# Four experts' expansions on one core: Strassen's scheme for two slices, two blocks of d_model and two halves of a tile's tokens

## The reference

```python
def _moe2_ref(x, domain_probs, w1, w2):      # x 1536 x 384, w1 4 x 384 x 1024, w2 4 x 1024 x 384
    p = domain_probs / (domain_probs.sum(-1, keepdims=True) + 1e-09)
    out = np.zeros((N, D), dtype=np.float32)
    for e in range(E):
        h = np.maximum(x @ w1[e], 0.0)
        out += p[:, e:e + 1] * (h @ w2[e])
    return out
```

## Time and profile before

| | |
|---|---|
| median of 3 runs | 681.5 us (680.98 to 681.69) |
| profiled execution | 681.51 us, span 679.7 us |
| granted TensorE clock | 1.0 of full |
| TensorE busy | 670.0 us (99%) |
| VectorE, ScalarE, GpSimd busy | 267.6, 182.4, 163.1 us |
| expert stage, from the first relu to the last matmul's start | 271.35 to 675.62 us |

### The profile page before, as it was taken

One profiled execution on the slowest core, in us unless ns is written; L12 is line 12 of the kernel. 1 busy time (PEld: TensorE's weight loads), 2 busy tenths in 40 slices (PEclk: granted clock), 3 DMA queues, 4 the chain that ended last, 5 costly groups with the idle time before them and its releaser, 6 DMA issues.

```text
span 679.7 us, 10802 instructions
## 1 busy us (share of the span) xinstructions
PE 670.0 (99%) x4251; PEld 589.1 (87%) x4251; DVE 267.6 (39%) x462; ACT 182.4 (27%) x351; POOL 163.1 (24%) x173
## 2 busy tenths in 40 slices
PE   9999999999999999999999999999999999999997
PEld 6888899877778888899999999999999999999997
DVE  7888878765634333212121212121212121212122
ACT  3663444433435444211111111111111111111110
POOL 3888322222001666400025400026300000000000
PEclk9999999999999999999999999999999999999999
DMA  9913322220001332100013100013100000001011
GB/s 342 405 60 124 118 83 87 79 82 1 1 1 42 96 96 94 46 1 1 0 47 94 47 0 0 0 47 95 45 1 0 0 1 0 1 1 46 0 47 47
DMA packets 12857, 38.74 MB, mean 57 GB/s; under 512 B 1552, under 2 KB 3344, under 8 KB 12816
## 3 DMA queue, kind: packets, MB, share of 16 engines
q1 hardware_dynamic: 12528, 37.77, 16.2%
q10 hardware_dynamic: 288, 0.39, 0.2%
HBM read 35.80 MB, written 2.36 MB: 56 GB/s over the span
## 4 chain that ended last, share of the span: by engine, by line
PE 91%; DVE 5%; ACT 1%; issue 1%; POOL 1%; DVEq 0%; ACTq 0%; POOLq 0%
PE bank L909 29%; PE bank L911 28%; PE bank L910 28%; PE bank L799 2%; PE bank L878 1%; DVE fr L546 1%; PE bank L856 1%; DVE fr L538 1%; PE bank L825 1%; DVE w_lo L630 1%; PE bank L811 1%; PE bank L868 1%; DVE bank L665 0%; DVE x_lo L622 0%; DVE g_lo L671 0%
## 5 line engine op out<-in xcount | busy, mean ns | idle before, releaser
L742 DVE SCALAR_TENSOR_TENSOR g_lo<-bank,g_hi 128x512 fp32r<-128x512 f32 x96 | 66.4, 692 | 308.4 <-ACT g_hi L506 308.4
L909 PE MATMUL bank<-x_lo,w_hi 128*128 128x512 f32 (+2 forms) x480 | 182.0, 379 | 1.7 <-DVE x_lo L622 0.9
L911 PE MATMUL bank<-x_hi,w_hi 128*128 128x512 f32 (+2 forms) x480 | 178.6, 372 | 0.0
L910 PE MATMUL bank<-x_hi,w_lo 128*128 128x512 f32 (+2 forms) x480 | 177.3, 369 | 0.0
L506 ACT ACTIVATE g_hi<-bank 128x512 fp32r<-128x512 f32 x96 | 57.5, 599 | 340.9 <-PE bank L911 340.9
L911 PE MATMUL bank<-w_hi,g_hi 128*128 128x384 f32 x384 | 129.7, 338 | 0.0
L910 PE MATMUL bank<-w_hi,g_lo 128*128 128x384 f32 x384 | 129.6, 337 | 0.0
L909 PE MATMUL bank<-w_lo,g_hi 128*128 128x384 f32 x384 | 129.3, 337 | 0.0
L911 PEld LDWEIGHTS bank<-x_hi,w_hi 128*128 128x128 f32 x480 | 90.1, 188 | 17.6
L909 PEld LDWEIGHTS bank<-x_lo,w_hi 128*128 128x128 f32 x480 | 90.1, 188 | 17.2 <-issue 1.8
L910 PEld LDWEIGHTS bank<-x_hi,w_lo 128*128 128x128 f32 x480 | 90.3, 188 | 12.7
(11 more groups left out here) (71 smaller groups left out, 545.4 us busy)
## 6 DMA issues: line engine op xcount, KB each, us to landing
raw<-w_dram SPq DMA_DIRECT2D x48, 384.0 KB, 3.1
rkw<-rkw_dram SPq DMA_DIRECT2D x10, 772.5 KB, 4.4
tok<-tok_dram SPq DMA_DIRECT2D x12, 576.0 KB, 4.2
out_dram<-acc SPq DMA_DIRECT2D x10, 192.0 KB, 1.9
rkw<-rkw_dram SPq DMA_DIRECT2D x2, 512.0 KB, 4.4
rkw<-rkw_dram SPq DMA_DIRECT2D x2, 260.5 KB, 3.4
out_dram<-acc ACTq DMA_DIRECT2D x2, 192.0 KB, 2.3
u_rep<-u_dram SPq DMA_DIRECT2D x1, 192.0 KB, 6.2
```

The source lines that it names most:

```text
L742: dve.scalar_tensor_tensor(out=g2[1][:, r, :], in0=p_h[j % 2][:, :], scalar=0.0, in1=g2[0][:, r, :].bitcast(F32), op0=ALU.max, op1=ALU.sub ...
L909: pe.matmul(out, wh, ml, start=start, stop=False)
L910: pe.matmul(out, wl, mh, start=False, stop=False)
L911: return pe.matmul(out, wh, mh, start=False, stop=stop)
```

## The change

A pair of slices (hidden rows 1 and 2) by the first two of three blocks of d_model, times those two blocks of x by two halves of 256 tokens, is a 2 x 2 by 2 x 2 block product. It is now computed with seven block products in place of eight (Winograd's form), of the blocks and of sums of them on either side. The third block of d_model is added as before, over all 512 tokens.

- **TensorE** (`up2`, per pair): P1 and P6 into the halves of bank 6, P7 and P5 into those of bank 7, then the third block's product for both slices into banks 0 and 1, onto which the last three products are added: two on bank 0 (one a half) and one on the first half of bank 1. `down_pair` contracts both slices of the pair before.
- **ScalarE** copies P1 and P5 to SBUF (`copy_products`) ahead of the pair's two relus.
- **VectorE** (`combine`) adds up what the four blocks of the result need, in banks 0 and 1, ahead of the two lo parts.
- **GpSimd** forms four sums of weight blocks for each pair (`split`) and four sums of x's blocks for each tile, once (`token_sums`), and splits them all into hi and lo parts.
- **Space**: slots 0 to 3 of the weights' arrays hold the sums of six pairs, slots 4 to 15 six pairs of slices (before: eight pairs). `acc` and `g2` move to where the first stage's arrays lie; the sums of tokens and copies get room behind them.

Lines that only open semaphores and some waits are left out, as are unchanged lines.

```diff
@@ -54,6 +54,14 @@
+QUARTER = TILE // 2
+PAIRS2 = J2 // 2
+NPAIR = NE * PAIRS2
+SUMS = 4
+FREE = SUMS * P * 6 // (2 * DM)
+RING2 = (J1 - FREE) // 2
@@ -138,9 +146,15 @@
-            sb("beside_g1", [P, 2 * TILE + 2 * RING1 * TILE], scope=scope)
...
+            xt_hi = sb("xt_hi", [P, NT * SUMS * QUARTER], F32R, scope=scope)
+            with ExitStack() as inner:
+                xt_raw = sb("xt_raw", [P, NT * SUMS * QUARTER], scope=inner)
+            xt_lo = sb("xt_lo", [P, NT * SUMS * QUARTER], F32R, scope=scope)
+            x_whole = sb("x_whole", [P, 2, 2, QUARTER], scope=scope)
+            u_sum = sb("u_sum", [P, 3, QUARTER], scope=scope)
+            p_copy = sb("p_copy", [P, 2, QUARTER], scope=scope)
@@ -235,7 +256,11 @@
         def slot_of(e, j):
-            return e % 2 * J2 + j
+            return FREE + (e * PAIRS2 + j // 2) % RING2 * 2 + j % 2
+        def sums_of(t, g):
+            return t[:, 0:FREE, :].rearrange("p s c -> p (s c)")[:, g % RING2 * SUMS * P:(g % RING2 + 1) * SUMS * P]
@@ -287,11 +312,11 @@
             def load_expert_slice(e, j):
-                slot = slot_of(e, j)
-                if e < 2:
+                slot, used = slot_of(e, j), e * PAIRS2 + j // 2 - RING2
+                if used < 0:
...
-                    sp.wait_ge(s_down, STEP1 + (e - 1) * (NT * J2) - J2 + j + 1 + RING)
+                    sp.wait_ge(s_down, STEP1 + used // PAIRS2 * (NT * J2) + (NT - 1) * J2 + used % PAIRS2 * 2 + 2 + RING)
...
@@ -380,14 +405,57 @@
-            def split(e, j):
-                slot = slot_of(e, j)
-                pool.wait_ge(s_raw[slot], 16 * (e // 2 + 2))
-                pool.tensor_copy(w_hi[:, slot, :], raw[:, slot, :]).then_inc(s_wp, 1)
-                pool.wait_ge(s_wp, e * J2 + j + 1)
-                pool.tensor_tensor(w_lo[:, slot, :], raw[:, slot, :], w_hi[:, slot, :].bitcast(F32),
+            def split(g):
+                e, q = g // PAIRS2, g % PAIRS2
+                slots = slot_of(e, 2 * q), slot_of(e, 2 * q + 1)
+                for slot in slots:
+                    pool.wait_ge(s_raw[slot], 16 * (g // RING2 + 2))
+                a11, a12 = raw[:, slots[0], 0:P], raw[:, slots[0], P:2 * P]
+                a21, a22 = raw[:, slots[1], 0:P], raw[:, slots[1], P:2 * P]
+                s1, s2, s3, s4 = (sums_of(raw, g)[:, i * P:(i + 1) * P] for i in range(SUMS))
+                pool.tensor_tensor(s1, a21, a22, ALU.add).then_inc(s_ws, 1)
+                pool.tensor_tensor(s3, a11, a21, ALU.subtract).then_inc(s_ws, 1)
...
+                pool.tensor_tensor(s2, s1, a11, ALU.subtract).then_inc(s_ws, 1)
...
+                pool.tensor_tensor(s4, a12, s2, ALU.subtract).then_inc(s_ws, 1)
+                for slot in slots:
+                    pool.tensor_copy(w_hi[:, slot, :], raw[:, slot, :]).then_inc(s_wp, 1)
...
+                pool.tensor_copy(sums_of(w_hi, g), sums_of(raw, g)).then_inc(s_wp, 1)
+                for i, slot in enumerate(slots):
...
+                    pool.tensor_tensor(w_lo[:, slot, :], raw[:, slot, :], w_hi[:, slot, :].bitcast(F32),
+                                       ALU.subtract).then_inc(s_w, 1)
...
+                pool.tensor_tensor(sums_of(w_lo, g), sums_of(raw, g), sums_of(w_hi, g).bitcast(F32),
...
+            def token_sums(T):
+                pool.wait_ge(s_py, NC)
+                pool.wait_ge(s_x2, KT + (T + 2) * KT)
+                cols = slice(T * TILE, (T + 1) * TILE)
+                for k in range(2):
+                    pool.tensor_tensor(x_whole[:, k, :, :].rearrange("p h t -> p (h t)"), x_hi[:, k, cols].bitcast(F32),
+                                       x_lo[:, k, cols].bitcast(F32), ALU.add).then_inc(s_xq, 1)
+                first = T * SUMS * QUARTER
+                t1, t2, t3, t4 = (xt_raw[:, first + i * QUARTER:first + (i + 1) * QUARTER] for i in range(SUMS))
...
+                pool.tensor_tensor(t1, x_whole[:, 0, 1, :], x_whole[:, 0, 0, :], ALU.subtract).then_inc(s_xq, 1)
...
+                pool.tensor_tensor(t3, x_whole[:, 1, 1, :], x_whole[:, 0, 1, :], ALU.subtract).then_inc(s_xq, 1)
...
+                pool.tensor_tensor(t2, x_whole[:, 1, 1, :], t1, ALU.subtract).then_inc(s_xq, 1)
...
+                pool.tensor_tensor(t4, x_whole[:, 1, 0, :], t2, ALU.subtract).then_inc(s_xq, 1)
...
+                sums = slice(first, first + SUMS * QUARTER)
+                pool.tensor_copy(xt_hi[:, sums], xt_raw[:, sums]).then_inc(s_xq, 1)
...
+                pool.tensor_tensor(xt_lo[:, sums], xt_raw[:, sums], xt_hi[:, sums].bitcast(F32),
+                                   ALU.subtract).then_inc(s_xt, 1)
@@ -417,9 +485,15 @@
-            for e in range(NE):
-                for j in range(J2):
-                    split(e, j)
+            token_sums(0)
+            for g in range(PAIRS2):
+                split(g)
+            token_sums(1)
+            for g in range(PAIRS2, RING2):
+                split(g)
+            token_sums(2)
+            for g in range(RING2, NPAIR):
+                split(g)
@@ -500,20 +574,36 @@
-            def hi_relu(n, j):
-                act.wait_ge(s_up, n + 1)
-                act.wait_ge(s_down, n + 1)
-                act.activation(g2[0][:, j % RING, :], p_h[j % 2][:, :], ACT.Relu).then_inc(s_gh, 1)
-            for j in range(LAG):
-                hi_relu(STEP1 + j, j)
+            def hi_relu(i, p, o):
+                act.wait_ge(s_c, i * 4 + 2 * o + 2)
+                act.wait_ge(s_down, i * 2 + (STEP1 + o + 1))
+                act.activation(g2[0][:, p % 2 * 2 + o, :], bank[o][:, :], ACT.Relu).then_inc(s_gh, 1)
+            def copy_products(i):
+                act.wait_ge(s_p, i * 4 + 1)
+                need(act, s_c, i * 4 - 3)
+                act.copy(p_copy[:, 0, :], bank[6][:, 0:QUARTER]).then_inc(s_pc, 1)
+                act.wait_ge(s_p, i * 4 + 2)
+                need(act, s_c, i * 4 - 1)
+                act.copy(p_copy[:, 1, :], bank[7][:, QUARTER:TILE]).then_inc(s_pc, 1)
+            def pair(i, p):
+                copy_products(i)
+                for o in range(2):
+                    hi_relu(i, p, o)
+            pair(0, 0)
             for m in range(KT):
...
-            for j in range(LAG, J2):
-                hi_relu(STEP1 + j, j)
+            for p in range(1, PAIRS2):
+                pair(p, p)
...
-                for j in range(J2):
-                    hi_relu(it * J2 + (STEP1 + j), j)
+                for p in range(PAIRS2):
+                    pair(it * PAIRS2 + p, p)
@@ -736,12 +826,41 @@
-            def lo_relu(n, j):
-                r = j % RING
-                dve.wait_ge(s_gh, n + (1 - STEP1))
-                dve.scalar_tensor_tensor(out=g2[1][:, r, :], in0=p_h[j % 2][:, :], scalar=0.0,
-                                         in1=g2[0][:, r, :].bitcast(F32), op0=ALU.max,
-                                         op1=ALU.subtract).then_inc(s_g, 1)
+            def combine(i):
+                p1, p5 = (p_copy[:, k, :] for k in range(2))
+                p6 = bank[6][:, QUARTER:TILE]
+                c11, c12, c22 = bank[0][:, 0:QUARTER], bank[0][:, QUARTER:TILE], bank[1][:, QUARTER:TILE]
+                u2, u3, u4 = (u_sum[:, k, :] for k in range(3))
+                def twice(ap):
+                    return ap.unsqueeze(1).broadcast_to([P, 2, QUARTER])
+                def in_halves(ap):
+                    return ap.rearrange("p (h t) -> p h t", h=2)
+                dve.wait_ge(s_pc, i * 2 + 1)
+                dve.tensor_tensor(u2, p1, p6, ALU.add).then_inc(s_u2, 1)
+                dve.wait_ge(s_pc, i * 2 + 2)
+                dve.wait_ge(s_u2, i * 2 + 1)
+                dve.tensor_tensor(u_sum[:, 1:3, :], in_halves(bank[7][:, :]), twice(u2), ALU.add).then_inc(s_u2, 1)
+                dve.wait_ge(s_p, i * 4 + 3)
+                dve.tensor_tensor(c11, p1, c11, ALU.add).then_inc(s_c, 1)
+                dve.wait_ge(s_u2, i * 2 + 2)
+                dve.tensor_tensor(c12, c12, u4, ALU.add).then_inc(s_c, 1)
+                dve.wait_ge(s_p, i * 4 + 4)
+                dve.tensor_tensor(c22, p5, c22, ALU.add).then_inc(s_c, 1)
+                dve.wait_ge(s_c, i * 4 + 3)
+                dve.tensor_tensor(in_halves(bank[1][:, :]), in_halves(bank[1][:, :]), twice(u3), ALU.add).then_inc(s_c, 1)
+            def lo_relu(i, p):
+                for o in range(2):
+                    r = p % 2 * 2 + o
+                    dve.wait_ge(s_gh, i * 2 + o + 1)
+                    dve.scalar_tensor_tensor(out=g2[1][:, r, :], in0=bank[o][:, :], scalar=0.0,
+                                             in1=g2[0][:, r, :].bitcast(F32), op0=ALU.max,
+                                             op1=ALU.subtract).then_inc(s_g, 1)
@@ -763,14 +882,15 @@
             def tile(e, T, first=False):
...
-                base = e * (NT * J2) + T * J2 + STEP1
-                for j in range(LAG, J2 + LAG):
-                    if j < J2 or not end:
-                        lo_relu(base + j, j)
```

(120 more changed lines are left out.)

## The result

The changed kernel takes 666.19 us (median of 6 runs, 666.10 to 666.61), the one before 681.13 us (6 runs) beside it: ratio 0.978, 95% interval 0.9767 to 0.9793. That is 14.9 us less; 666.5 us had been forecast, within 665.0 to 670.1.

The account below looks back on a forecast made before the run. TensorE's streamed columns were taken as the bound. From 681.5 us, 15.6 us came off (325 ns for each of 48 pairs) and 0.6 us was added for group starts: 666.5 us, eight-in-ten range 665.0 to 670.1.

Parts of the forecast that it names:

- The bound: Expert stage: TensorE's matmuls fill the 4.194 us per slice without a gap, so only columns streamed through it can be saved.
- The price of a 256-column matmul: TensorE's expansion: 117.5 ns each with a new weight load, against 231.9 ns for 512 columns.
- The saving per pair: TensorE: 12 matmuls of 512 go, 21 of 256 come, one return goes: 325 ns, 15.6 us over 48 pairs.
- three group starts: Extra semaphore-guarded starts in TensorE's expansion, per pair: 4 ns each, 12 ns a pair, 0.6 us in all.
- the return: TensorE's switch from contraction back to expansion: one of two per pair goes, saving 10 ns.
- the tail behind the last matmul: End of the kernel, after TensorE's last matmul: stays as before.
- The rival of bound loads: TensorE's 256-column matmuls come 188 ns apart, each load passing before the next: 71 us more, 738 us; chance 2%.
- Registers: TensorE's 256-column matmuls with register addresses, in half the pairs: no cost taken.
- The upper bound of 5.5 ns a matmul: TensorE's register instructions run just in time, 123 ns against 117.5: 2.8 us in all; within a 9% rival.
- The chain: ScalarE's and VectorE's copies, additions, relus and lo parts hide behind the previous pair's contraction: no cost; late-chain rival 5%.
- the point where the gain is gone: Late-chain rival, TensorE stopping at bank 0 or 1 every pair: gain eaten at 2.7 us longer chain; chance 5%.
- GpSimd: Weight sums and splits: 9.9 us a pair, least margin 13 us, no cost; rival of being late once 2%.

Follow-up runs that it names:

- seven copies: Changed kernel with seven more 256-column ScalarE copies in every pair, each waiting for the one before, ahead of the first relu: 670.71 us, ratio 0.9846.
- the last experiment: Changed kernel with four more subtractions of 768 columns on GpSimd in every pair: 679.55 us, ratio 0.9973 to the kernel before.
- eleven copies: Changed kernel with eleven more 256-column ScalarE copies in every pair, each waiting for the one before, ahead of the first relu: 750.42 us, ratio 1.101.

## Why the prediction was right

- **The bound.** TensorE's columns were the bound before, and are after. Taking away a product takes away its time (one product fewer: 17.7 us), and taking away the Strassen scheme alone gives the old time back (1.0001).
- **The price of a 256-column matmul** was the step on which it hung. I took 117.5 ns from the earlier trace rows; the 21 in a pair came 118.8 ns apart in the mean. That gives 26 ns a pair, or 1.3 us.
- **The saving per pair** was forecast as 325 ns less 12 ns for group starts, 313 ns; it was 300. Against 117.5 and 231.9 ns a matmul the expansion cost 28 ns more, where I had taken 12 for three group starts. It does not lie at those three: the pair's first three intervals are 11 ns over, the last nine 16, and the nine between them together are not over at all. The contractions became 14 ns shorter, where I had 10 for the return. The sum, 15.0 us, met 14.9, but the last 0.5 us of that is luck: inside the stage 14.4 were saved, and the tail behind the last matmul, which I had put down as unchanged, gave 0.5 to 0.7.
- **The rival of bound loads** (738 us) fell: the 256-column matmuls start 118 to 119 ns apart with a load of 188 ns each, over stretches of 36 in a row too. The Trainium skill's sentence that a load overlaps matmuls only when its row group differs ("TensorE: Matmul & The Clock Gate", Part 3) does not hold for these loads. The gap of N / 2.4 + 2.5 ns of the same page of the Trainium skill (Part 2, on the back-to-back gap) gave an estimate of 14.3 us, nearer to the 14.4 of the stage than my 15.0. That is luck: both its widths are low by 7 to 8% against the traces, and in the difference this cancels.
- **Registers.** Nothing, as taken. The upper bound of 5.5 ns a matmul was far off: with and without them a pair takes 8.087 us.
- **The chain.** I had its second lo part end at 7.2 to 7.7 us; it ended at 6.99, mainly since VectorE's additions start 0.34 us apart though each row is 0.42 long. It costs nothing as long as it hides behind the contraction of the pair before. The room was larger than the 2.5 and 2.4 us that I gave, 3.4 and 3.2, mainly as the 0.5 us that I had added for register instructions did not appear. Copies of 1.7 us in all cost nothing, 3.0 us cost only behind the drains and at the very end, 4.8 us cost 84 us. What I had not priced was the tile end: I said that the drains end before the next pair needs VectorE, which is so by 0.2 us (405.25 + 2.26 against 407.72), so a longer chain pushes the drains into that pair's sums, and there it is felt first. I had put the point where the gain is gone at 2.7 us of a longer chain. With seven copies the second lo part ends 2.5 us later than in the changed kernel, and 10.5 us of the gain are still there; with eleven all of it is gone.
- **GpSimd.** 8.8 us a pair against 9.9, as its operations start about 0.05 us before the one before has ended by its row, where I had added gaps. It had 18 us to spare, not 13.

## What to carry to other kernels

When TensorE is the bound, trading columns for additions pays as long as the added work hides behind matmuls that were there anyway. Halving the columns of a matmul, with a fresh load each, cost 3.5 ns for each added matmul here, at 256 columns; nothing narrower was run. Before making such a trade, write the chain of the added work against the clock of one period and find where it is due; the room is smallest where a periodic extra (here the drains) sits on the same engine. A late helper can cost more than its wait: behind both waits of the last experiment (4.5 and 5.4 us) TensorE worked at half rate for a while.

## What the runs showed that was not expected

- Behind a wait of 4.5 us TensorE ran on at 0.12 us per 256 columns for about 0.8 us, and only then at 0.21, until 302.0; behind one of 5.4 us it ran at 0.21 from the start. With intervals of 2.2 to 2.8 us in the run with eleven copies the clock fell behind seven inside the stage and not behind the other five; behind those of 1.4 us or less never.
- A GpSimd subtraction of 768 columns whose two inputs are the same took 1.47 us in the median (1.51 in the stretch shown), with two different ones 1.85. The output's type, which differs too, hardly matters: at 512 columns 1.29 us into fp32 (L441) and 1.30 into fp32r (L432).
- A wait of TensorE costs 0.1 us beyond itself, in the interval behind it.
- The tail behind the last matmul was 0.5 to 0.7 us shorter in all seven traces with Strassen's products than in the three without. What links the two is not shown.
